# Perceptron first layers in seven block products per pair of weight tiles

## The reference, cut to what matters

```python
# block 1: mixes tokens, then channels
h = np.maximum(xt @ w_tok1, 0.0) @ w_tok2
u = x + h.transpose(0, 2, 1)
x = u + np.maximum(u @ w_ch1, 0.0) @ w_ch2            # 512 -> 1536 -> 512
# block 2: real part of a 2-D FFT, layer norm, channels
u = x + np.real(np.fft.fft(np.fft.fft(x, axis=1), axis=2))
un = (u - mu) / np.sqrt(var + 1e-06)
out = u + np.maximum(un @ w_ch1, 0.0) @ w_ch2          # 512 -> 2048 -> 512
```

## Time and profile before

| | |
|---|---|
| median of 3 runs | 603.35 us (603.11 to 604.53) |
| the profiled execution, its own time | 603.05 us |
| its span in the profile | 601.2 us |
| share of the span busy: PE, DVE, ACT, POOL | 99%, 48%, 31%, 10% |

### The profile page before, as it was taken

How to read it: one execution, slowest core, us unless ns; L and a number is a source line. 1 busy time by engine, 2 the same in 40 slices (tenths; PEclk the granted TensorE clock), 3 DMA queues, 4 the chain that set the end, 5 groups by cost and what they waited for, 6 DMA issues and landing times.

```text
span 601.2 us, 8473 instructions
## 1 busy us (share of the span) xinstructions
PE 595.3 (99%) x3512; PEld 541.3 (90%) x3512; DVE 285.9 (48%) x494; ACT 187.6 (31%) x333; POOL 61.8 (10%) x106
## 2 busy tenths in 40 slices
PE   8999999999999999999999999999999999999997
PEld 6999889899999999999989999999899999999996
DVE  7987665333432682336567623556432522332223
ACT  6676123232432332222233332223322222222220
POOL 6884000300000020000002000000000000000000
PEclk9999999999999999999999999999999999999999
DMA  8790320321232221121121212121222122221302
GB/s 312 275 342 29 105 71 8 103 71 69 79 103 70 71 67 39 36 70 36 70 70 37 70 36 71 35 71 36 70 71 65 40 71 70 71 70 38 139 0 106
DMA packets 24567, 49.04 MB, mean 82 GB/s; under 512 B 3021, under 2 KB 3921, under 8 KB 24529
## 3 DMA queue, kind: packets, MB, share of 16 engines
q1 hardware_dynamic: 23808, 46.69, 23.1%
q0 software_dynamic: 576, 1.72, 1.0%
q10 hardware_dynamic: 144, 0.10, 0.1%
HBM read 45.35 MB, written 3.15 MB: 81 GB/s over the span
## 4 chain that ended last, share of the span: by engine, by line
PE 97%; DMA 1%; DVE 1%; SPq 1%; issue 0%
PE banks L780 28%; PE banks L779 28%; PE banks L778 28%; PE banks L842 4%; PE banks L802 2%; PE banks L850 2%; PE banks L836 2%; DMA qTs<-qT_dram 1%; PE banks L861 1%; PE banks L863 1%; PE banks L868 1%; PE banks L790 1%; DVE u L630 1%; PE banks L810 0%; PE banks L923 0%
## 5 line engine op out<-in xcount | busy, mean ns | idle before, releaser
L780 PE MATMUL banks<-uth,wh 128*128 128x384 f32 x448 | 150.3, 336 | 0.0
L778 PE MATMUL banks<-uth,wl 128*128 128x384 f32 x448 | 150.3, 336 | 0.0
L779 PE MATMUL banks<-utl,wh 128*128 128x384 f32 x448 | 150.0, 335 | 0.0
L780 PE MATMUL banks<-wh,hh 128*128 128x512 f32 x336 | 132.0, 393 | 0.0
L779 PE MATMUL banks<-wl,hh 128*128 128x512 f32 x336 | 131.9, 393 | 0.0
L778 PE MATMUL banks<-wh,hl 128*128 128x512 f32 x336 | 131.6, 392 | 0.0
L469 DVE TENSOR_TENSOR wl<-raw,wh 128x1024 fp32r<-128x1024 f32 x56 | 68.4, 1224 | 128.5 <-ACT wh L316 128.2
L589 DVE SCALAR_TENSOR_TENSOR hl<-banks,hh 128x384 fp32r<-128x384 f32 x112 | 61.9, 556 | 92.1 <-ACT hh L436 92.0
L316 ACT ACTIVATE wh<-raw 128x1024 fp32r<-128x1024 f32 x56 | 59.2, 1059 | 139.2 <-PE banks L780 139.1
L436 ACT ACTIVATE hh<-banks 128x384 fp32r<-128x384 f32 x112 | 54.8, 491 | 141.2 <-PE banks L780 141.2
L778 PEld LDWEIGHTS banks<-uth,wl 128*128 128x128 f32 x448 | 84.1, 188 | 2.1
(11 more groups left out here) (154 smaller groups left out, 526.2 us busy)
## 6 DMA issues: line engine op xcount, KB each, us to landing
raw<-w1b_dram SPq DMA_DIRECT2D x32, 256.0 KB, 2.7
raw<-w2b_dram SPq DMA_DIRECT2D x32, 256.0 KB, 2.9
raw<-w1a_dram SPq DMA_DIRECT2D x24, 256.0 KB, 2.6
raw<-w2a_dram SPq DMA_DIRECT2D x24, 256.0 KB, 2.9
kTs<-kT_dram SPq DMA_DIRECT2D x8, 384.0 KB, 6.0
qTs<-qT_dram SPq DMA_DIRECT2D x8, 384.0 KB, 6.9
kns<-kn_dram SPq DMA_DIRECT2D x8, 384.0 KB, 7.3
vns<-vn_dram SPq DMA_DIRECT2D x8, 384.0 KB, 4.6
```

The costliest lines, as they stand in the source:

```text
L778: mm(o, ll, rh_, start=start, stop=False)
L779: mm(o, lh, rl_, start=False, stop=False)
L780: return mm(o, lh, rh_, start=False, stop=stop)
```

## The change

Two tiles of hidden units are now made together, as a pair `p` (28 pairs, 6, 6, 8, 8 in the four chunks). The weights of a pair are a two by two matrix of blocks (two hidden tiles by two halves of the features, A11, A12, A21, A22), the features are blocks too (two halves of the features by two halves of the tokens, B11, B12, B21, B22). Instead of eight block products PE makes seven (Winograd's form of Strassen's algorithm) from sums of blocks, S1 to S4 of the weights and T1 to T4 of the features. One `product` is 6 matmuls of 384 columns.

What is added for it:
- POOL makes the weight sums of each pair (`combos`, 4 operations of 256 columns) and takes over the low part of the second layer's weights (`down_lo`, 2 of 512 columns).
- The products of a pair run through banks 6 and 7 only, partly on top of one another, so ACT copies bank 6 out three times in a pair (`snapshot`, 384 columns), and DVE adds bank 7 to each copy (`hidden_sum`, 384 columns). Relu and low part follow as before, three of four now from SBUF.
- Seven weight blocks instead of eight quarter tiles are split (`up_first_hi`/`_lo` with 512 and 256 columns, `up_second_hi`/`_lo` with 768 and 256).
- Each transposed tile is done in two units, "x" (tokens of the first half) and "y" (second half): four transposes each, then `block_x_hi`, `block_x_lo`, `block_sums` (4 operations of 256 columns on DVE, two of them with a wait for the one before), `block_y_hi` with two further copies of 512 columns on ACT, `block_y_lo`, and on POOL `sums_lo` (2 of 512 columns).
- The memory is laid out anew. There is one buffer of raw first-layer weights (`raw1`) and one of second-layer weights (`raw2`), where a ring of three stood.

In a pair PE goes through the twelve `down` pieces of the pair before (n = 0 to 11, three matmuls of 512 columns each) with the seven products and up to six side units between them. The loop on PE, the ACT and DVE loops, and what they call:

```diff
+FOURIER = {2: (("d1", 0), ("d1", 1), ("d1", 2), ("d1", 3), ("d1", 4), ("q", 0)),
+           3: (("p", 0), ("q", 1), ("p", 1), ("q", 2), ("p", 2), ("p", NA)),
+           4: BLOCKS[0]}
+SIDE = [{1: BLOCKS[0], 2: BLOCKS[1], 3: BLOCKS[2]},
+        {**FOURIER, 5: (None, None, ("x", 1), ("y", 1), ("x", 2), ("y", 2))},
+        {**FOURIER, 5: BLOCKS[1], 6: BLOCKS[2]}, {}]
+FIRST_BLOCKS = ((4, 5), (6, 7), (0, 1))
+SIDE_BANK = (7, 7, 6, 7, 6, 7)
...
+            def combos(p):
+
+                pool.wait_ge(s_w1, 16 * (p + 1))
+                if p:
+                    pool.wait_ge(blo_ready, p)
+                a11, a12, a21, a22 = [raw1[:, i, k * 2 * L:(k + 1) * 2 * L] for i in range(2) for k in range(2)]
+                nc.gpsimd.tensor_tensor(sraw[:, RS1, :], a21, a22, ALU.add).then_inc(combo_step, 1)
+                pool.wait_ge(combo_step, p + 1)
+                minus(sraw[:, RS2, :], sraw[:, RS1, :], a11).then_inc(combos_ready, 1)
+                minus(sraw[:, RS3, :], a11, a21)
+                pool.wait_ge(combos_ready, 2 * p + 1)
+                minus(sraw[:, RS4, :], a12, sraw[:, RS2, :]).then_inc(combos_ready, 1)
+
+            def down_lo(p, i):
+                pool.wait_ge(w2h_ready, 2 * p + i + 1)
+                minus(w2l[:, i, :], raw2[:, i, :], f(w2h[:, i, :])).then_inc(w2l_ready, 1)
+
+            def sums_lo(target, n):
+                e, b, t = event(target, n), target % B, TILES[target][n]
+                cols = slice(t * L, (t + 1) * L)
+                for i, k in enumerate((T2, T1)):
+                    pool.wait_ge(sum_hi, 2 * e + i + 1)
+                    minus(tl[b][:, k:k + 2, :, cols], ts[b][:, k - T2:k - T2 + 2, :, cols],
+                          f(th[b][:, k:k + 2, :, cols])).then_inc(sum_lo, 1)
+
...
+            def block_x_hi(target, n, src):
+                e, b, t = event(target, n), target % B, TILES[target][n]
+                act.wait_ge(tr_done, 2 * e + 1)
+                if target >= 2:
+                    act.wait_ge(y_added, 4 * (b + 1))
+                copy(ts[b][:, T3 - T2, :, t * L:(t + 1) * L], src[:, 0:FH].rearrange("p (k t) -> p k t", k=2))
+                copy(th[b][:, B11:B21 + 1, :, t * L:(t + 1) * L],
+                     src[:, :].rearrange("p (s k t) -> p s k t", s=2, k=2)).then_inc(block_hi, 1)
+
+            def block_y_hi(target, n, src):
+                e, b, t = event(target, n), target % B, TILES[target][n]
+                cols = slice(t * L, (t + 1) * L)
+                act.wait_ge(sums_ready, 2 * e + 2)
+                copy(th[b][:, B22, :, cols], src[:, FH:DM].rearrange("p (k t) -> p k t", k=2)).then_inc(block_hi, 1)
+                for k in (T2, T1):
+                    copy(th[b][:, k:k + 2, :, cols], ts[b][:, k - T2:k - T2 + 2, :, cols]).then_inc(sum_hi, 1)
...
+            for p in range(NP):
+                ch, j = place(p)
+                fourier = ch in (1, 2)
+                if p:
+                    down_hi(p - 1, 1)
+                snapshot(p, 0)
+                act.wait_ge(x_ready, 3 * p + 1)
+                if p:
+                    act.wait_ge(down_done, 12 * (p - 1) + 3)
+                relu_hi(h0h[:, first], snap[:, 0, :])
+                snapshot(p, 1)
...
+                relu_hi(h1h[:, p % 2, second], snap[:, 2, :])
+                up_first_hi(p + 1)
+                act.wait_ge(prod_done, 7 * p + 6)
+                relu_hi(h1h[:, p % 2, first], bank[6][:, 0:HALF])
+                down_hi(p, 0)
+                if fourier and j == 1:
+                    fold_hi(ch - 1, 1)
+                act.wait_ge(x_ready, 3 * p + 3)
+                if p:
+                    act.wait_ge(down_done, 12 * (p - 1) + 6)
+                relu_hi(h0h[:, second], snap[:, 1, :])
+                side_hi(ch, j, 2)
+                side_hi(ch, j, 3)
+                up_second_hi(p + 1)
+                if fourier and j == 0:
+                    edge_row(ch - 1)
+                if fourier and j == 1:
+                    fold_hi(ch - 1, 2)
+                side_hi(ch, j, 4)
+                side_hi(ch, j, 5)
...
+            def block_sums(target, n, x, y):
+
+                e, b, t = event(target, n), target % B, TILES[target][n]
+
+                def part(k):
+                    return ts[b][:, k - T2, :, t * L:(t + 1) * L]
+
+                x2, y1, y2 = [z.rearrange("p (k t) -> p k t", k=2) for z in (x[:, FH:DM], y[:, 0:FH], y[:, FH:DM])]
+                dve.wait_ge(tr_done, 2 * e + 2)
+                link(minus(part(T1), y1, part(T3)))
+                link(minus(part(T2), y2, part(T1)))
+                minus(part(T4), x2, part(T2)).then_inc(sums_ready, 1)
+                minus(part(T3), part(T2), part(T3)).then_inc(sums_ready, 1)
...
+            def ln_stats(b, n):
+
+                t = TILES[2][n]
+                dve.wait_ge(y_added, 4 * (b + 1))
+                for i in range(2):
+                    link(nc.vector.bn_stats(stats[:, NA * i + t, :], u[:, NC * b + NA * i + t, :]))
+                    link(nc.vector.bn_aggr(mv[:, b, t, i, :], stats[:, NA * i + t, :]))
+                nc.vector.tensor_scalar(veps[:, b, t, :], mv[:, b, t, :, 1], 1e-6, None, ALU.add).then_inc(ve_ready, 1)
...
+            def hidden_sum(p, n, i, done):
+
+                dve.wait_ge(prod_done, 7 * p + done)
+                dve.wait_ge(snap_ready, 3 * p + i + 1)
+                nc.vector.tensor_tensor(snap[:, i, :], bank[7][:, 0:HALF], snap[:, i, :], ALU.add).then_inc(x_ready, 1)
+                dve.wait_ge(x_ready, 3 * p + n)
+
+            first, second = slice(0, HALF), slice(HALF, S)
+            for p in range(NP):
+                ch, j = place(p)
+                fourier = ch in (1, 2)
+                if fourier and j == 1:
+                    fold_sum(ch - 1, 0)
+                hidden_sum(p, 1, 0, 2)
+                hidden_lo(p, 1, h0l[:, first], snap[:, 0, :], h0h[:, first])
...
+                if fourier and j == 4:
+                    ln_stats(ch - 1, 0)
+                if fourier and j == 5:
+                    ln_norm(ch - 1, 1, 0)
+                    ln_norm(ch - 1, 1, 1)
...
+                hidden_sum(p, 2, 2, 5)
+                hidden_lo(p, 2, h1l[:, p % 2, second], snap[:, 2, :], h1h[:, p % 2, second])
...
+                up_first_lo(p + 1)
+                if fourier and j == 4:
+                    ln_norm(ch - 1, 0, 0)
+                    ln_norm(ch - 1, 0, 1)
+                hidden_lo(p, 3, h1l[:, p % 2, first], bank[6][:, 0:HALF], h1h[:, p % 2, first])
+                hidden_sum(p, 3, 1, 7)
+                hidden_lo(p, 4, h0l[:, second], snap[:, 1, :], h0h[:, second])
...
+                side_lo(ch, j, 2)
+                side_lo(ch, j, 3)
+                up_second_lo(p + 1)
...
+                if fourier and j == 4:
+                    ln_stats(ch - 1, 1)
+                    ln_stats(ch - 1, 2)
+                if ch == 1 and j == 5:
+                    ln_norm(ch - 1, 2, 0)
+                    ln_norm(ch - 1, 2, 1)
+                side_lo(ch, j, 4)
+                side_lo(ch, j, 5)
...
+            def product(p, a, t, o, start):
+                b = place(p)[0] % B
+                for k in range(2):
+                    cols = slice(k * L, (k + 1) * L)
+                    mm(o[:, 0:HALF], al[:, a, cols], th[b][:, t, k, :], start=start and k == 0, stop=False,
+                       skip_group_check=True)
+                    mm(o[:, 0:HALF], ah[:, a, cols], tl[b][:, t, k, :], start=False, stop=False, skip_group_check=True)
+                    last = mm(o[:, 0:HALF], ah[:, a, cols], th[b][:, t, k, :], start=False, stop=(k == 1),
+                              skip_group_check=True)
+                last.then_inc(prod_done, 1)
...
+            for t in (0, 3, 1, 4, 2, 5):
+                token_mix(0, t)
+            for n in range(NA):
+                token_mix(1, n)
+                for i in range(2):
+                    block_transpose(0, n, i, bank[FIRST_BLOCKS[n][i]])
+            token_mix(1, 3)
+
+            for p in range(NP):
+                ch, j = place(p)
+                down(p - 1, 0)
+                pe.wait_ge(alo_ready, p + 1)
+                if j == 0:
+                    pe.wait_ge(block_lo, 2 * event(ch, NA) - 1)
+                bank_read(p, 6)
+                product(p, A11, B11, bank[6], True)
+                down(p - 1, 1)
+                bank_read(p, 7)
+                product(p, A12, B21, bank[7], True)
+                if p == 0:
+                    token_mix(1, 4)
+                down(p - 1, 2)
+                pe.wait_ge(snap_ready, 3 * p + 1)
+                if j == 0:
+                    pe.wait_ge(sum_lo, 2 * event(ch, NA) - 1)
+                product(p, S2, T2, bank[6], False)
+                side(p, 0)
+                if p == 0:
+                    token_mix(1, 5)
+                down(p - 1, 3)
+                down(p - 1, 4)
+                side(p, 1)
+                pe.wait_ge(snap_ready, 3 * p + 2)
```

(43 more changed lines are left out.)

880 lines of the change are left out of this document (483 added, 397 removed).

## The result

The changed kernel takes 626.75 us (median of 4 runs, 626.3 to 628.94) where the kernel before takes 603.25 beside it: ratio 1.039, 95% interval 1.036 to 1.042. It is slower by 23.5 us; forecast were 9, from 594 to 620. The profiled execution has a span of 625.2 us, 24.0 more than before.

A forecast was written before the change was run, and what follows sets the result against it. PE, busy 99%, was taken to bound the kernel. 603.05 less 29.1 us of removed matmuls plus 38.5 of new waits gave 612.4, forecast as a median of 612.5 us, slower by 1.5%; range 594 to 620.

The forecast's parts named there:

- Removed, 29.1 us: On PE, each of 28 pairs has 42 matmuls of 384 columns where it had 48, saving 29.1 us.
- Plain pair, 15.57 without waits: A pair without side work takes 15.57 us of PE time, every ACT, DVE and POOL answer covered, so no wait.
- Opening: Before the first product, PE waits 5.2 us while ACT and DVE hand the tiles' blocks to and fro.
- first `down`: The first `down` waits 2.9 us for POOL, which clears `e1raw` and issues four DMAs before making the low weights.
- S3: In the pair after the fifth, chunks 1 and 2, S3 waits 3.6 us behind DVE's work; 1.0 more if always met.
- End of chunk 1: Before the last "x" of chunk 1, PE waits 7.0 us for the chain through DVE and ACT.
- chunk 0: In pairs with transposes, the next pair's first snapshot comes 2.0, 1.2 and 0.7 us late on ACT, 3.8 together.
- third pairs: In the third pairs of chunks 1 and 2, a bank is used again 0.5 us before it is read.
- last pairs of chunk 2: No wait was forecast for these pairs.
- From 32.9 (free) to 43.5 (always met) I take 38.5: Sum of PE's waits: 32.9 us if DVE and POOL share SBUF freely, 43.5 if they exclude each other; 38.5 taken.
- PE's clock: Rival: the clock halves behind the new gaps, adding 5 to 10 us, 617 to 622; chance 0.16.
- The rival that the products win: ACT and DVE run ahead, waits sum to less than 27 us, kernel faster, mostly 585 to 600; chance 0.26.

The follow-up runs named there:

- e5: Changed kernel with the product of S1 and T1 made twice in every pair, so PE has all 3512 matmuls again: 651.69 us, ratio 1.080.
- e9: e4 with POOL kept occupied by memsets that read nothing, ahead of each combo and `down_lo`: 618.41 us, ratio 1.025.
- e4: Changed kernel with POOL's `combos` and `down_lo` on 8 columns in place of 256 and 512 after the first pair: 614.44 us, ratio 1.016.
- e12: Changed kernel with useless matmuls on PE ahead of all four long waits, the opening's in a bank free at once: 619.6 us, ratio 1.027.
- e1: Changed kernel with useless matmuls on PE ahead of its four longest waits; the opening's waited for a bank and started 2.9 us late: 623.04 us, ratio 1.033.
- e2: Changed kernel, chunks 1 and 2: second `ln_stats` ahead of `up_second_lo`, third behind the next pair's first `hidden_lo`: 618.34 us, ratio 1.025.
- e3: Changed kernel, last pair of chunk 1: the third tile's two `ln_norm` moved ahead of the second tile's `block_x_lo` and `block_sums`: 625.69 us, ratio 1.037.
- e6: Changed kernel, reordered in chunks 1 and 2: `ln_stats` one by one, chunk 1's norms early, third tile ahead of `up_second_hi` and `_lo`: 614.76 us, ratio 1.018.
- e10: e8 with three more order edits: second half's `down_hi`, sixth and seventh pairs' `ln_norm`, and fold operations moved later: 625.92 us, ratio 1.039.
- e8: Changed kernel with the order edits of e6 and e7 together: 610.23 us, ratio 1.011.
- e13: e8 with the e10 edits that gained, 11 matmuls ahead of the first product, and POOL's `sums_lo` behind the next pair's `combos`: 614.32 us, ratio 1.020.
- e7: Changed kernel, reordered in the opening and chunk 0: next tile's "x" first on ACT, first `down_hi`, `down_lo`, second `combos` before `e1raw`'s clearing: 622.17 us, ratio 1.030.

## Why the prediction was wrong

**Removed, 29.1 us:** right as a count, 168 matmuls. e5 puts 25 on it in time, in part because the fold pairs gain nothing.

**Plain pair, 15.57 without waits:** 15.65 in chunk 3, with no wait; right, but for 0.08 in each pair, 2.3 in all.

**Where the waits are:** mostly right, and the releasers too but for one. Opening: 5.2 forecast, 4.39 seen; first `down` 2.9, seen 2.24, with POOL's low weights ready 0.1 ahead of it; but I had POOL late by clearing `e1raw` and by its DMAs, and it waited for ACT's `down_hi`, so the size is near by luck. S3: 3.6 to 4.6, seen 4.72 twice. End of chunk 1: 7.0, seen 6.65. Second pairs: 1.4 to 5.0, seen 1.9 and 2.2. Too small were chunk 0 (3.8, seen 7.1), the third pairs (0.5, seen 2.2, of which 1.3 is one gap: their first snapshot stands behind `down_hi` and the third fold; the rest was not traced) and the last pairs of chunk 2 (nothing, seen 2.1, none in e9).

**The step that failed first: "From 32.9 (free) to 43.5 (always met) I take 38.5".** e4 and e9 show 10.8 us for `combos` and `down_lo` alone, where the upper bound had 10.6 with `sums_lo`: in sum the cost is that of "always met". Not place by place, though: the two S3 waits grew by 1.07 each as forecast (1.0), the fold pairs by 1.5 and 1.8, not 3.6; what I missed are the pair ends of chunks 0 and 2, 1.1 each. The step was 5 us short or more.

**The second: PE's clock, which I kept apart as a rival with 0.16 and 5 to 10 us.** It is no other case but a part of this one: each long gap of the forecast sum carries its slow stretch. e12 has 7.2 us. The price stood on no row of the kernel before: the 3.5 us of slow work behind each gap were an assumption, and 2.9 to 5.7 were seen. But a term that I could price should not have been put at nothing in the sum while the gaps were in it.

612.5 + 5 + 7.2 is 624.7, and with the 2.3 of the pairs 627, where 626.75 was measured. That it closes so well is partly luck: the places above differ by some us in both directions.

**The rival that the products win** was refuted, and by no small amount: it needed waits under 27, and PE's waits are 36 by the trace, 53 us with the clock and the longer pairs. The one that DVE and POOL "never meet" fell with e9.

What stays open: what decides whether the clock falls behind a gap of 1.9 to 3.7 us, and what the 0.8 us of the third pairs beyond their gap are.

## What to carry to other kernels

An engine that is at 99% is at the bound only because everything else is early; work taken off it is worth its time only where the others stay early, so walk the pairs with the most side work first. Every gap of 4.3 us and more on TensorE cost the gap and slow matmuls behind it here, and those from 1.9 us on did in some executions: put both in the sum. Before moving an operation back in a list, ask when its own result is wanted, not only who stands behind it.

## What was not expected of the hardware

The length of a gap does not tell whether PE's clock falls behind it. The wait ahead of the first `down` is 2.24 us in eight executions. Behind it the matmuls went at full pace in the changed kernel, e1, e4 and e5, and at half in e2, e3, e6 and e9. Windows of the changed kernel and then of e2, right behind it, in the columns as above:

```profile
113.60:116.60 3.00, 3.00 (x15) 2.74 (x16) 2.25 (x3) 2.29 (x5) 1.13 (x1) 1.00 0.39 87
```

```profile
112.45:115.45 3.00, 3.00 (x9) 2.71 (x10) 2.31 (x3) 1.73 (x4) 1.19 (x1) 0.50 0.25 87
```

So too with others: it fell behind gaps of 1.93 (e10), 1.96 (e6) and 2.81 (e8, nine matmuls of 384 columns 0.32 apart), and did not behind 1.95 (e8), 2.83 and 3.66 (e13). Behind all 25 gaps of 4.3 us and more that follow the token mixing in these traces it fell. The slow stretch varies as well: behind the same wait of 4.7 in chunk 2 it was 2.9 us in e7 and 5.7 in the changed kernel.

Half a gap filled is not a gap halved: in e1, 2.9 us of idling and then 18 matmuls gave slow matmuls among these. And POOL operations of 512 columns that meet DVE cost both, 2.02 in place of 1.29 on POOL and, with two of them in turn, 3.29 in place of 1.29 on DVE (the rows at 303.31 and 302.31), so work given to an idle GpSimd is not free for VectorE.
